# The order of the first stage of a fused attention and two-layer kernel: a weight product ahead of the scores, loads by need, a scale moved behind a matmul, V stored by pairs

## The reference, cut to what matters

```python
# 8 batches, 8 heads, S=512 tokens, 32 states, D=64; all float32
a  = softmax(x @ state.T / 8)            # each token over the states
xread = a @ state
a2 = softmax(state @ x.T / 8)            # each state over the tokens
sread = a2 @ x
X = rows of concat([xread, sread], tokens)     # 4608 x 512
h = (X @ w1) * (X @ w2) @ w3 @ w_out           # w1, w2: 512x1024, w3: 1024x1024, w_out: 1024x512
out = tanh_shrink(h @ w_in2) @ w_out2          # h - tanh(h), 2048 wide
```

## Time and profile before

| | us |
|---|---|
| three runs, median (lowest to highest) | 1308.58 (1307.06 to 1311.42) |
| the profiled execution, device time | 1306.28 |
| its span, first to last instruction | 1304.5 |
| PE busy in the span | 1257.1 |
| DVE busy, ACT busy | 811.1, 572.4 |

### The profile page before, as it was taken

One profiled execution on the slowest core, in us unless ns is written; L12 is line 12 of the kernel. 1 busy time (PEld: TensorE's weight loads), 2 busy tenths in 40 slices (PEclk: granted clock), 3 DMA queues, 4 the chain that ended last, 5 costly groups with the idle time before them and its releaser, 6 DMA issues. The chain is left out here.

```text
span 1304.5 us, 17417 instructions
## 1 busy us (share of the span) xinstructions
PE 1257.1 (96%) x6408; PEld 1028.6 (79%) x6408; DVE 811.1 (62%) x1340; ACT 572.4 (44%) x1067; POOL 16.0 (1%) x14
## 2 busy tenths in 40 slices
PE   5898799999999999999999999999999999999997
PEld 3666587888888888878888888888888888888886
DVE  4777635444444443388767667676676676776765
ACT  3555534333444343355534444444344444443443
POOL 0111000000000000000000000000000000000000
PEclk9999899999999999999999999999999999999999
DMA  7688764213332321032100100100001001000000
GB/s 265 235 248 302 192 148 130 81 56 106 106 105 70 108 80 64 16 97 65 56 10 17 49 1 17 49 17 31 18 16 48 0 16 48 14 32 10 8 33 17
DMA packets 63376, 97.28 MB, mean 75 GB/s; under 512 B 5200, under 2 KB 38992, under 8 KB 59344
## 3 DMA queue, kind: packets, MB, share of 16 engines
q1 hardware_dynamic: 60576, 91.25, 22.3%
q10 hardware_dynamic: 2736, 5.24, 1.2%
HBM read 61.87 MB, written 34.60 MB: 74 GB/s over the span
## 5 line engine op out<-in xcount | busy, mean ns | idle before, releaser
L1356 ACT ACTIVATE hq<-bank 128x512 f32<-128x512 f32 (+1 forms) x144 | 82.8, 575 | 397.3 <-PE bank L1459 397.1
L1413 DVE TENSOR_TENSOR hw<-hw,hq 128x512 f32<-128x512 f32 (+1 forms) x144 | 95.5, 663 | 198.0 <-ACT hw L1361 194.5
L1459 PE MATMUL bank<-ysp_hi,wi_hi 128*128 128x512 f32 (+1 forms) x576 | 217.3, 377 | 0.7 <-DVE ysp_lo L1154 0.7
L1459 PE MATMUL bank<-ysp_lo,wi_hi 128*128 128x512 f32 (+1 forms) x576 | 217.3, 377 | 0.0
L1459 PE MATMUL bank<-ysp_hi,wi_lo 128*128 128x512 f32 (+1 forms) x576 | 217.2, 377 | 0.0
L1481 PE MATMUL wide<-wz_hi,gsp_hi 128*128 128x512 f32 x544 | 212.7, 391 | 4.1 <-DVE gsp_lo L1407 3.2
L1481 PE MATMUL wide<-wz_lo,gsp_hi 128*128 128x512 f32 x544 | 211.8, 389 | 0.0
L1481 PE MATMUL wide<-wz_hi,gsp_lo 128*128 128x512 f32 x544 | 211.7, 389 | 0.0
L1459 PEld LDWEIGHTS bank<-ysp_hi,wi_hi 128*128 128x128 f32 x576 | 108.3, 188 | 21.6 <-DVE ysp_lo L1154 1.1
L1459 PEld LDWEIGHTS bank<-ysp_lo,wi_hi 128*128 128x128 f32 x576 | 108.2, 188 | 20.4
L1459 PEld LDWEIGHTS bank<-ysp_hi,wi_lo 128*128 128x128 f32 x576 | 108.4, 188 | 20.2
(11 more groups left out here) (129 smaller groups left out, 1830.3 us busy)
## 6 DMA issues: line engine op xcount, KB each, us to landing
v_dram<-vs SPq DMA_DIRECT2D x128, 128.0 KB, 2.6
vr<-v_dram SPq DMA_DIRECT2D x64, 256.0 KB, 2.9
xs<-in_x_rows SPq DMA_DIRECT2D x8, 1024.0 KB, 6.6
y_dram<-ysb SPq DMA_DIRECT2D x8, 1024.0 KB, 4.3
yr<-y_dram SPq DMA_DIRECT2D x32, 256.0 KB, 3.4
out<-ysb SPq DMA_DIRECT2D x8, 1024.0 KB, 4.6
xT<-in_x_cols SPq DMA_DIRECT2D x7, 1024.0 KB, 7.8
w3r<-in_w_cols SPq DMA_DIRECT2D x8, 512.0 KB, 4.5
```

The lines of the kernel that those rows point to most:

```text
L1356: act.activation(hq[:, f % 2, 0:w], ph[f % 2][:, 0:w], ACT.Square).then_inc(sq_done, 1)
L1413: dve.tensor_tensor(u, u, q, ALU.mult).then_inc(w2_done, 1)
L1459: mm = pe.matmul(ph[f % 2][:, 0:w], wi[s][:, c, f * P:(f + 1) * P], ysp[k][u][c][:, 0:w], start=c + m == 0, stop=c == KC - 1 and m == LAST)
```

## The change

Six edits, all in the front but the last. (1) PE does pieces 0 and 1 first, then the first scores, and the turns and the read of entry 0 between pieces 2 to 6; SP loads w3 and w_out first, x in one DMA behind half of w_out, and the states in two parts. (2) The weights a2 stay unscaled: DVE's two multiplications an entry go, `a2_turn` waits for the exponent instead, and `copy_sr` becomes two activations, one a head, with the inverse as scale. (3) `copy_srT(e-1)` stands ahead of `tokens_max(e)` on DVE. (4) Splits of the states and of w1 and w2 move within the entries: `split_s` ahead of `copy_sr`, and in entries 6 and 7 one half of a quarter at a time. (5) V is stored by pairs of units, 1 MB in four DMAs of 32 rows by 8 KB; two places of a pair until unit 11, three from unit 12 on (the third where w3 stood). (6) In moe1 the last four splits of the first batch's V stand behind the first steps, not ahead of them.

In the diff, the loop from `LATE + 1` is that of ACT and the one with `copy_srT` that of DVE; the last two pieces, of moe1, stand alike on ACT and DVE.

```diff
-RING = 4
+RING = 3
+FIRST_SPLITS = (4, 6, 8, 9, 11, 12, 13, 15, 16)
...
-        def store(v):
+        def store(m):
             for k in range(2):
-                sp.wait_ge(emptied[k], turn_of["v", v] + 1)
-            q, i, c = of_unit(v)
+                sp.wait_ge(emptied[k], turn_of["v", 2 * m + 1] + 1)
+            q, i, c = of_unit(2 * m)
...
+    def slot(m):
+        return m % 2 if m < FIRST[LATE + 1] // 2 else m % 3
+    def stored(m):
+        return 64 * sum(slot(n) == slot(m) for n in range(m))
...
-        load_xT(sp, 0, ((0, 1), (2, 3)))
         load_w3(sp, 0)
-        for n in range(NF1 // 2):
-            sp.dma_start(wor[:, 2 * n:2 * n + 2, :], wo_v[:, 2 * n:2 * n + 2, :]).then_inc(wo_in[n], 16)
+        load_wo(0)
+        load_wo(1)
+        load_xT(sp, 0)
+        load_wo(2)
+        load_wo(3)
+        load_w3(sp, 1)
         load_xs(sp, 0)
-        load_w3(sp, 1)
+        sp.dma_start(sT[:, 1:B, :, :], state_cols[:, 1:B, :, :]).then_inc(sT_in[1], 16)
...
         def copy_sr(e):
             act.wait_ge(sread_done, e + 1)
+            act.wait_ge(tok_inv, e + 1)
             after(act, sr_turned, e)
-            act.activation(sr[:, :], ps[:, 0:P], ACT.Copy).then_inc(sr_copied, 1)
+            for g in range(G):
+                act.activation(sr[:, g * D:(g + 1) * D], ps[:, g * D:(g + 1) * D], ACT.Copy, scale=tinv[:, g:g + 1]).then_inc(sr_copied, 1)
...
         for e in range(LATE + 1, B):
...
             exp_a2(e)
+            if e == B - 1:
+                split_w(2, 1)
             turn_a(e - 1)
+            split_s(v // 4 + 1)
...
             unit(v + 2)
+            split_w(e - LATE + 1, 0)
             copy_sr(e)
             unit(v + 3)
-            for u in range(2):
-                split_w(e - LATE + 1, u)
-            split_s(v // 4 + 1)
...
-        def tokens_scale(e):
+        def tokens_invert(e):
             dve.wait_ge(tok_exp, 2 * e + 2)
+            after(dve, sr_copied, 2 * e)
...
-            for g in range(G):
-                dve.tensor_scalar(a2[:, g, :], a2[:, g, :], tinv[:, g:g + 1], None, ALU.mult).then_inc(a2_ready, 1)
...
         for e in range(1, LATE + 1):
             v, p = FIRST[e], first_piece(e)
+            copy_srT(e - 1)
             tokens_max(e)
-            copy_srT(e - 1)
...
         def a2_turn(e):
-            pe.wait_ge(a2_ready, 2 * e + 2)
+            pe.wait_ge(tok_exp, 2 * e + 2)
...
-        scores(0)
-        scores_turn(0)
         piece(0)
         piece(1)
-        a2_turn(0)
+        scores(0)
         piece(2)
         piece(3)
+        scores_turn(0)
+        piece(4)
+        piece(5)
+        a2_turn(0)
+        piece(6)
         sread(0)
-        for p in range(4, EARLY):
-            piece(p)
...
-                    split_v(b + 1, f)
+                    if isinstance(b, int) and b == 0:
+                        for n in range(FIRST_SPLITS[f], FIRST_SPLITS[f + 1]):
+                            split_v(n // NF1, n % NF1)
+                    else:
+                        split_v(b + 1, f)
...
-        for f in range(VRING, NF1):
-            split_v(0, f)
         entry(0, 0)
```

More of the change, by code:

```diff
@@ L79 @@
 EARLY = 7
+V_STORED = (7 * 64, 6 * 64, 3 * 64)
+V_STORED_HALF = (6 * 64, 6 * 64, 2 * 64)
 class Map:
@@ L132, in build @@
         room_d = Map(nc, vr_at, end)
-        vr = second("vr", [P, VRING, G, 2, P])
+        vr = second("vr", [P, VRING, 2, G, P])
         prod_hi, prod_lo = sem("prod_hi"), sem("prod_lo")
@@ L146, in prefetch_v @@
         def prefetch_v(sp):
-            half = UNITS - 4
             for m in range(RING):
-                sp.wait_ge(v_stored[m], 64 * half // RING)
+                sp.wait_ge(v_stored[m], V_STORED_HALF[m])
             for f in range(VRING):
@@ L172, in build @@
                 place = third_small if (n, f) == (1, NF1 - 1) else third_high
-                vsp[n].append(place(f"vsp{n}_{f}", [P, G, 2, P], F32R))
+                vsp[n].append(place(f"vsp{n}_{f}", [P, 2, G, P], F32R))
         ahead = (aT, aTs, vr, vsp, v_in_sems, aT_hi, aT_lo, v_hi, v_lo)
@@ L268, in stage_front @@
     quarter(room_d, 1)
-    vs = room_d("vs", [P, RING, G, W])
+    vs = [room_d(f"vs{n}", [P, G, 2, W]) for n in range(2)]
     wos_at = room_d.at
@@ L300, in stage_front @@
     ident_zeroed, ident_ready = sem("ident_zeroed"), sem("ident_ready")
-    sT_in, xT_in, xs_in = sem("sT_in"), sem("xT_in"), sem("xs_in")
+    sT_in, xT_in, xs_in = [sem(f"sT_in{n}") for n in range(2)], sem("xT_in"), sem("xs_in")
     w_in, w_hi, w_lo = [[sem(f"w_in{k}{u}") for u in range(2)] for k in range(KC)], sem("w_hi"), sem("w_lo")
@@ L417, in sync @@
             piece(p)
-            store(v)
+            stores(v + 1)
             piece(p + 1)
             piece(p + 2)
-            store(v + 1)
+            stores(v + 2)
             piece(p + 3)
@@ L426, in sync @@
             load_xs(sp, e + 1)
-            if v + 2 < FIRST[e + 1]:
-                store(v + 2)
+            stores(FIRST[e + 1])
             if e == 1:
@@ L436, in sync @@
                 load_xT(sp, e + 1)
-            for n in range(3):
-                store(v + n)
+            stores(v + 3)
             if e + 1 < B:
                 load_xs(sp, e + 1)
-            store(v + 3)
-        for v in range(FIRST[B], UNITS):
-            store(v)
+            stores(v + 4)
+        stores(UNITS)
     def gpsimd(pool):
@@ L482, in split_s @@
             if g == 0:
-                act.wait_ge(sT_in, 16)
+                for n in range(2):
+                    act.wait_ge(sT_in[n], 16)
             q, i, _ = of_unit(4 * g)
@@ L493, in unit @@
             act.wait_ge(filled[0], turn_of["v", v] + 1)
-            after(act, v_out[v % RING], 64 * (v // RING))
-            act.activation(vs[:, v % RING, 0, :], pair("v", v)[0], ACT.Copy).then_inc(emptied[0], 1)
+            after(act, v_out[slot(v // 2)], stored(v // 2))
+            act.activation(vs[slot(v // 2)][:, 0, v % 2, :], pair("v", v)[0], ACT.Copy).then_inc(emptied[0], 1)
         def copy_st(e):
@@ L566, in scalar @@
             piece(p + 4)
+            if e in (1, 3, 5):
+                split_s((e + 1) // 2)
+            if e in (2, 3):
+                split_w(1, e - 2)
             copy_sr(e)
@@ L641, in unit @@
             dve.wait_ge(filled[1], turn_of["v", v] + 1)
-            after(dve, v_out[v % RING], 64 * (v // RING))
-            dve.tensor_copy(vs[:, v % RING, 1, :], pair("v", v)[1]).then_inc(emptied[1], 1)
+            after(dve, v_out[slot(v // 2)], stored(v // 2))
+            dve.tensor_copy(vs[slot(v // 2)][:, 1, v % 2, :], pair("v", v)[1]).then_inc(emptied[1], 1)
         def turn_a2_half(e):
@@ L708, in vector @@
         split_w3(1)
+        rows_max(0)
+        tokens_invert(0)
+        rows_sub(0)
+        piece(3)
+        turn_a2_half(0)
         rows_sum(0)
-        for p in range(3, EARLY):
-            piece(p)
+        split_s(0)
         for u in range(2):
             split_w(0, u)
-        split_s(0)
+        piece(6)
         rows_invert(0)
```

85 lines of the change are left out of this document (43 added, 42 removed).

## The result

The changed kernel takes 1293.8 us (median of four runs, 1292.2 to 1294.45) beside 1309.11 (1307.06 to 1311.42) for the kernel before: a ratio of 0.9881, with a 95% interval of 0.9862 to 0.99. Its profiled execution is 1293.56 with a span of 1291.8, 12.7 shorter than before.

What follows compares the result with a forecast made beforehand. PE bounds where it has pieces; in entries 6 and 7 DVE's and ACT's order does. Terms 6.0 + 3.5 + 1.0 + 1.7 = 12.2 off 1306.28 give 1294.1, 1296.4 on the median's scale; forecast 1295, range 1287 to 1302.

Steps and rivals of the forecast that it cites:

- signs of being wrong: Trace signs against the forecast, such as scores 7 waiting for x by more than 2 or a start gap over 5.
- A: The start and entry 1: earlier first pieces, fewer waits and less slow clock win 6.0 us (4 to 7).
- Now PE's first work needs 0.5 MB: At the start: 0.5 MB each of w3 and w_out lets piece 0 begin at 9.2; 3.2 won by scores 1.
- B: Entries 2 to 5: copying srT ahead of the maxima removes PE's waits; 3.5 us won (2.5 to 3.95).
- PE's idle 3.95 is all srT: Entries 2 to 5: all of PE's idle 3.95 us is waiting for DVE's copy of the turned read.
- C: Entries 6 and 7 and the units behind: scaling gone and splits reordered, less late x and slow clock; 1.0 (-1 to 4).
- 1.85 for the other half: Entries 6 and 7: DVE waits 1.85 us on ACT for the other half of quarter 2 of w.
- 0.7 late (0 to 1.5): Entry 7: x lands 0.7 us late because a 1 MB pair stands in its queue where 0.5 MB did.
- D: First step of moe1: ACT's splits no longer stand ahead of it; 1.7 us won (1.5 to 1.9).
- At nothing: Parts forecast to win nothing: two-piece read copy, the scaling in entries 0 to 5, and the paired stores.
- R3: Rival: paired stores of V block the emptying of units and all behind it; not faster, 1317 us; chance 0.07.
- R4: Rival: at the start the first loads crawl and piece 2 waits as before; start gives 2, 1300 us; chance 0.07.

Runs made afterwards that it cites:

- the version put together: Changed kernel with pieces 0 to 3 in a row, quarter 3 of w loaded behind x of entry 7, two moves of w splits: 1280.61 us, ratio 0.9792 to before.

## Why the prediction was right, and where it was not

The time was 1293.8 for a forecast of 1295 (the profiled execution 1293.56 for a sum of 1294.1). The sum was nearer than its terms, since they missed on both sides, by 0.55 to 0.9 each; that it came within 0.6 is luck. One of the prediction's own signs of being wrong came true: scores 7 waited for x by 4.3, more than its 2.

*A, 6.0 forecast, 5.23 measured.* The steps stood as walked: piece 0 at 9.17 (9.2), a gap of 3.77 (3.8), scores 1 at 31.40 (30.7), sr waiting 1.22 (1.4), entry 1 16.45 (16.5). What was missing is in the slow clock behind the gap: some twelve matmuls, not seven, stood 0.43 apart, 2.4 and not 1.4. (In the three runs with scores 1 at 29.83 to 30.28 it was six or seven.) The prediction read from a gap of 2.45 that the clock can hold; the kernel before with moe1's splits alone has 2.46 at the same place, and there the next matmul took 0.80, at half clock. But the credit was wrong. "Now PE's first work needs 0.5 MB" was to win 3.2 by scores 1; the old order with the new loads gets there 1.6 sooner and to scores 2 3.2 sooner. Smaller loads and the moved copies and splits won A, and the pieces' place gave part of it back: the wait for sr, 1.22 against 0.19, and the work at half clock behind the gap.

*B, 3.5 forecast, 4.39 measured.* srT's waits are all gone. "PE's idle 3.95 is all srT" took the last releaser for the cause: with only srT put back the entries lose 1.8. The rest, as far as rows go, was DVE late behind a split of w that waited for ACT, and that edit I had costed in C alone. The 0.44 above the idle time is not in the waits: scores 4 took 1.53 before, where the other three entries, and all four now, have 1.09. The trace does not say why.

*C, 1.0 forecast, 0.45 measured.* The walk of DVE was right, 37.6 forecast and 36.9 measured once x is early; its longest wait for ACT, "1.85 for the other half", is 1.87. The term mis-sized is the lateness of x: "0.7 late (0 to 1.5)", where the wait for it was 4.3 and cost 3.25 of the stretch. I priced the pair of 1 MB in its queue, and the pair is worth 0.44; quarter 3, 1 MB that stood ahead of x before as well, I did not price. Why x landed 13.1 after scores 6 before and 15.2 even with single stores stays open: same order of issues, and more bytes moved before it landed (5.41 MB in 15.5 us against 5.98 in 17.6). The slow clock at the start of s1 (1.2) did not come in this kernel; eight of the twelve kernels of the experiments pay 0.7 to 2.0 for it. Its ground, "some 3.5 of work in the last 7", does not decide it: PE had 3.63 in the changed kernel, and 3.61 with the scaling put back, where s1 starts at half clock.

*D, 1.7 forecast, 2.6 measured,* of which 2.0 come with this edit alone. 0.6 more appears in every variant of the changed kernel and not there; 0.5 of it are waits on gsp_lo in the last stage (3.1 against 2.6). What they have to do with the front I did not find out.

*At nothing:* the scaling beside pieces, right (0.02 in entries 2 to 5), and the stores, right: no wait of PE on them, no time in the pairs. With twice as many stores the kernel took 1294.08 against 1293.8. R3's block came only as 0.66 of DVE (and 0.15 of ACT) waiting once for a store, in no row of PE; in the version put together it is 1.8 and 1.3. R4's "wins nothing" holds for the order of the start, but its reason does not: the first loads did not crawl (piece 0 at 9.17), and what the order lost, it lost to the gap.

## What to carry to other kernels

A wait names who came last, not who made it late: follow the late engine one step further back, to what it stood for, before the gain is booked to one edit. A load that lands late hides the worth of all that is moved behind it, so move the loads in its queue that are needed later out of its way first. And an order that leaves a gap in TensorE's work is to be compared with one that has none: here four pieces in a row, with the splits placed to suit them, reached scores 2 some 5 and 8 us ahead of the two other orders (of the 8, up to 1.6 are the clock's).

## What was not expected of the hardware

The same 1 MB on the same queue took 7.8, 9.0, 10.4 and 11.0 us to land, by what stood around it. And s1, whose code is the same in all, took 31.8 us in some kernels and up to 33.75 in others, by how much of its start fell at half clock: as much as most of these edits are worth. The idle time just ahead doesn't tell which: an idle of 3.08 ended 0.90 ahead of s1 in the changed kernel, where the first 5 us of s1 stood at full clock, and an idle of 3.08 ended 0.89 ahead of it with the scaling put back, where the granted clock of these 5 us was 0.66.
